# Attention and two MLPs on one core: first loads by head, a mixed first score and value order, and moved weight casts

## The reference

```python
scores = cap * np.tanh(scale * np.matmul(q, k.transpose(0, 1, 3, 2)) / cap)
attn = np.exp(scores - np.max(scores, axis=-1, keepdims=True))
attn = attn / (np.sum(attn, axis=-1, keepdims=True) + 1e-09)
x = np.matmul(attn, v)          # 896 x 768 after the heads are put side by side
x = np.maximum(x @ w_in1, 0.0) ** 2 @ w_out1
h = x @ w_in2
return (h / (1.0 + np.exp(-h))) @ w_out2
```

## Time and profile before

| what | us |
|---|---|
| median of three runs | 550.55 |
| the profiled execution, its own time | 549.79 |
| its span, first to last instruction | 547.9 |
| PE busy | 535.4 (98%) |
| PEld busy | 442.6 (81%) |
| DVE busy | 376.1 (69%) |
| ACT busy | 261.3 (48%) |
| POOL busy | 82.1 (15%) |

### The profile page before, as it was taken

One profiled execution on the slowest core, in us unless ns is written; L12 is line 12 of the kernel. 1 busy time (PEld: TensorE's weight loads), 2 busy tenths in 40 slices (PEclk: granted clock), 3 DMA queues, 4 the chain that ended last, 5 costly groups with the idle time before them and its releaser, 6 DMA issues.

```text
span 547.9 us, 7096 instructions
## 1 busy us (share of the span) xinstructions
PE 535.4 (98%) x2626; PEld 442.6 (81%) x2626; DVE 376.1 (69%) x597; ACT 261.3 (48%) x403; POOL 82.1 (15%) x54
## 2 busy tenths in 40 slices
PE   6999999999999999999999999999999999999995
PEld 5333333799999999999998999999999999999895
DVE  2199999977778652676799855556855345568985
ACT  3988889054444322454444434444533144454230
POOL 0999999300000000000000000000000000000000
PEclk9999999999999999999999999999999999999999
DMA  7888540151112201411122024202111141020645
GB/s 159 219 235 199 147 110 2 57 135 58 45 33 72 63 1 57 135 58 38 40 63 57 17 59 135 59 10 68 47 54 34 59 134 36 23 78 15 118 63 85
DMA packets 82116, 42.16 MB, mean 77 GB/s; under 512 B 26784, under 2 KB 79008, under 8 KB 82080
## 3 DMA queue, kind: packets, MB, share of 16 engines
q1 hardware_dynamic: 77952, 40.32, 28.6%
q10 hardware_dynamic: 4096, 1.38, 1.3%
q0 software_dynamic: 32, 0.00, 0.0%
HBM read 38.93 MB, written 2.75 MB: 76 GB/s over the span
## 4 chain that ended last, share of the span: by engine, by line
PE 76%; DVE 14%; issue 4%; SPq 3%; DMA 1%; ACT 1%; DVEq 0%; ACTq 0%
PE banks L494 25%; PE banks L496 25%; PE banks L495 25%; DVE den L815 3%; SPq L301 2%; DVE w_hl L866 1%; DVE x_hi L825 1%; DVE rinv L820 1%; DVE att_o L823 1%; DVE y L946 1%; DVE den_r L812 1%; DVE qk_f L800 1%; DMA qk_raw<-in_k_dram 1%; DVE qk_f L796 1%; SPq L322 1%
## 5 line engine op out<-in xcount | busy, mean ns | idle before, releaser
L494 PE MATMUL banks<-x_hi,w_hl 128*128 128x448 f32 x384 | 140.7, 367 | 0.0
L495 PE MATMUL banks<-x_lo,w_hl 128*128 128x448 f32 x384 | 140.5, 366 | 0.0
L496 PE MATMUL banks<-x_hi,w_hl 128*128 128x448 f32 x384 | 140.5, 366 | 0.0
L494 PE MATMUL banks<-g_hi,w_hl 128*128 128x448 f32 x336 | 123.3, 367 | 0.7 <-DVE w_hl L866 0.7
L496 PE MATMUL banks<-g_hi,w_hl 128*128 128x448 f32 x336 | 123.0, 366 | 0.0
L495 PE MATMUL banks<-g_lo,w_hl 128*128 128x448 f32 x336 | 123.0, 366 | 0.0
L494 PEld LDWEIGHTS banks<-x_hi,w_hl 128*128 128x128 f32 x384 | 72.1, 188 | 7.6 <-issue 1.4
L496 PEld LDWEIGHTS banks<-x_hi,w_hl 128*128 128x128 f32 x384 | 72.1, 188 | 6.2
L495 PEld LDWEIGHTS banks<-x_lo,w_hl 128*128 128x128 f32 x384 | 72.1, 188 | 6.2
L861 DVE TENSOR_TENSOR w_hl<-w_raw,w_hl 128x768 fp32r<-128x768 f32 x32 | 32.5, 1016 | 57.4 <-ACT w_hl L640 57.3
L494 PEld LDWEIGHTS banks<-g_hi,w_hl 128*128 128x128 f32 x336 | 63.1, 188 | 7.0 <-DVE w_hl L866 1.4
(11 more groups left out here) (64 smaller groups left out, 549.5 us busy)
## 6 DMA issues: line engine op xcount, KB each, us to landing
w_raw<-in_moe_w_in_dram SPq DMA_DIRECT2D x32, 384.0 KB, 3.4
w_raw<-in_moe_w_out_dram SPq DMA_DIRECT2D x24, 512.0 KB, 5.3
qk_raw<-in_k_dram SPq DMA_DIRECT2D x48, 112.0 KB, 2.7
qk_raw<-in_q_dram SPq DMA_DIRECT2D x40, 112.0 KB, 2.8
v_t<-in_v_dram SPq DMA_DIRECT2D x24, 96.0 KB, 2.8
out_dram<-rows SPq DMA_DIRECT2D x40, 56.0 KB, 2.2
qk_raw<-in_q_dram ACTq DMA_DIRECT2D x8, 112.0 KB, 4.1
out_dram<-rows ACTq DMA_DIRECT2D x8, 56.0 KB, 2.8
```

The costliest lines, as they stand in the source:

```text
L494: pe.matmul(dst, hi[:, kk, :], mov_hi, start=start, stop=False, skip_group_check=onto)
L495: pe.matmul(dst, hi[:, kk, :], mov_lo, start=False, stop=False, skip_group_check=onto)
L496: return pe.matmul(dst, lo[:, kk, :], mov_hi, start=False, stop=stop, skip_group_check=onto)
```

## The change

It has five parts.

1. *Loads.* The first two pairs are loaded by head: SP issues those of the even heads and ACT those of the odd heads, for pair 0 keys, then queries, then the same for pair 1, with no wait between. ACT also issues two of the four first value transfers.
2. *Order in the lead.* On PE the outputs of pairs 0 and 1 are cut in two halves (`output_first`, `output_rest`) that stand between the score units of the next pair. The sums of pair 0 come after all scores of pair 2. The wait for `v_x` moves to the product that reads it. WARM goes from 17 to 14.
3. *GpSimd.* The loop over pairs becomes straight code.
4. *Weight casts on ACT.* The first two weight tiles are rounded after pairs 7 and 9, one each.
5. *Groups.* In `model`, the sums of weight blocks and the first two products' rests for group 1 move on DVE ahead of the adding up of results of group 0. On ACT the rounding for product 1 of group 1 moves ahead of `x_high`. The epsilon is added with a `tensor_scalar` in place of the `scalar_tensor_tensor`.

```diff
-    WARM = 17
+    WARM = 14
@@ SP
-            load_part(At(0, 0), 0, k_v, s_first_in[0])
-            sp.wait_ge(s_first_in[0], 4 * DMA)
-            load_part(At(0, 1), 0, k_v, s_qk_in[1])
-            load_v(0)
+            load_head(0, 0, k_v, 0, s_first_in[0])
+            load_head(0, 1, q_v, 0, s_first_in[1])
+            load_head(1, 0, k_v, 0, s_qk_in[1])
+            load_head(1, 1, q_v, 0, s_qk_in[1])
+            load_v(0, range(0, 2))
             load_v_x(0)
@@ POOL
-                for j in range(2):
+                for j in range(PAIRS):
                     add_units(At(0, j))
-                two_steps(pool, 2, PAIRS - 2, add_units)
@@ PE
+            def output_first(j):
+                ...
+                values(j, 0)
+                values(j, 1)
+            def output_rest(j):
+                pe.wait_ge(s_exp, 2 * j.n + 2)
+                values(j, 2)
+                ...
+                values(j, CW).then_inc(s_val, 1)
-            for j in range(PAIRS):
+            for u in range(C):
+                scores(At(0, 0), u)
+            for j in range(2):
+                scores(At(0, j + 1), 0)
+                output_first(At(0, j))
+                for u in range(1, CW):
+                    scores(At(0, j + 1), u)
+                output_rest(At(0, j))
+                scores(At(0, j + 1), CW)
+            sums(At(0, 0))
+            for j in range(3, PAIRS):
                 ...
@@ ACT
-            load_q(0, s_first_in[1])
+            load_head(0, 0, k_v, 1, s_first_in[0])
+            load_head(0, 1, q_v, 1, s_first_in[1])
+            load_head(1, 0, k_v, 1, s_qk_in[1])
+            load_head(1, 1, q_v, 1, s_qk_in[1])
+            for g in range(2, C):
+                ...
-            act.wait_ge(s_first_in[1], 4 * DMA)
-            load_q(1, s_qk_in[1])
             for j in range(PAIRS - 1):
                 weights(At(0, j))
-            for p in range(2):
-                tile_high(0, 0, p)
+                if j in (7, 9):
+                    tile_high(0, 0, (j - 7) // 2)
@@ DVE, finish
-                dve.scalar_tensor_tensor(den[:, :], part, eps_t[:, 0:1], part,
-                                         op0=ALU.add, op1=ALU.max).then_inc(s_den, 1)
+                dve.tensor_scalar(den[:, :], part, eps_t[:, 0:1], None, ALU.add).then_inc(s_den, 1)
@@ DVE, model
                         if g == 0:
+                            prod_low(layer, s, 1, 0)
+                            w_s1(layer, s, 1)
+                            w_s3(layer, s, 1)
+                            w_s2(layer, s, 1)
+                            prod_low(layer, s, 1, 1)
                             if s == 1:
                                 post_12_u2(layer, g)
-                            w_s1(layer, s, g + 1)
```

More of the change, by code:

```diff
@@ L186, in wait @@
                 eng.wait_ge(s, n)
-        def two_steps(eng, first, count, step):
-            assert count % 2 == 0
-            with eng.Fori(0, count // 2) as i:
-                step(At(i, first))
-                step(At(i, first + 1))
         def shifted(eng):
@@ L294, in _, with load_head, load_v @@
         def _(sp):
-            def load_part(j, n, src, done):
-                for h in range(2):
-                    for a in range(2):
-                        at = n * QB * D + BL * (1 - a)
-                        rp = slice(D * h + BL * a, D * h + BL * a + BL)
-                        sp.dma_start(qk_raw[j.par][rp, at:at + QB * D],
-                                     src[bass.ds(j.no, 1), h][0]).then_inc(done, DMA)
+            def load_head(j, n, src, h, done):
+                for a in range(2):
+                    at = n * QB * D + BL * (1 - a)
+                    rp = slice(D * h + BL * a, D * h + BL * a + BL)
+                    sp.dma_start(qk_raw[j % 2][rp, at:at + QB * D], src[j, h]).then_inc(done, DMA)
             def load_qk(j):
-                load_part(j, 0, k_v, s_qk_in[j.par])
-                load_part(j, 1, q_v, s_qk_in[j.par])
-            def load_v(part):
+                for n, src in enumerate((k_v, q_v)):
+                    for h in range(2):
+                        load_head(j, n, src, h, s_qk_in[j % 2])
+            def load_v(part, groups=range(C)):
                 first, last = V_PARTS[part], V_PARTS[part + 1]
-                for g in range(C):
+                for g in groups:
                     at = g * CW * D
@@ L355, in _ @@
                 sp.wait_ge(s_turned, 2 * (j - 1))
-                load_qk(At(0, j))
+                load_qk(j)
                 if j % 2 == 0:
@@ L470, in output @@
                 values(j, 1)
+            def output_rest(j):
                 pe.wait_ge(s_exp, 2 * j.n + 2)
                 values(j, 2)
+                if j.n in V_PARTS[0:2]:
+                    pe.wait_ge(s_v_x_in[V_PARTS.index(j.n)], 2 * XB * DMA)
                 values(j, CW).then_inc(s_val, 1)
+            def output(j):
+                output_first(j)
+                output_rest(j)
             pe.wait_ge(s_const, 1)
@@ L1121, in _ @@
                             post_21_u3(layer, g)
-                        if not last:
+                        if g == 1:
                             prod_low(layer, s, g + 1, 0)
@@ L1132, in _ @@
                             leave(layer, s, g, 1)
-                        if not last:
+                        if g == 1:
                             w_s2(layer, s, g + 1)
                             prod_low(layer, s, g + 1, 1)
-                        elif s == 0:
+                        elif last and s == 0:
                             tile_low(layer, 1, 0)
-                        elif layer == 0:
+                        elif last and layer == 0:
                             tile_low(1, 0, 0)
```

29 lines of the change are left out of this document (15 added, 14 removed).

## The result

The changed kernel takes 547.7 us (median of 6 runs, 546.39 to 548.9) against 550.65 us for the kernel before (6 runs, 549.63 to 551.4): a ratio of 0.9949, 95% interval [0.9935, 0.9964]. The forecast was 547.4, its range 545.9 to 549.4. The profiled execution of the changed kernel took 548.26 us (span 546.5), so the two profiled executions lie 1.53 us apart, while the medians lie 2.95 apart. Both differences have to be explained.

A forecast was written before the change was run, and what follows sets the result against it. It took attention to set the end, paced first by ACT, then by PE, plus two weight waits. Loads 0.75, order 1.0, GpSimd 0.4, casts 0.3 and groups 0.65 make 3.1 us: 550.55 - 3.1 = 547.4, range 545.9 to 549.4.

The forecast's parts named there:

- Loads, 0.75: Start of the kernel: loading by head starts PE's first scores at 7.8 in place of 8.55, gaining 0.75 us (0.35 to 1.1).
- S0: The start of PE's first scores: 8.55 us in the kernel before, forecast 7.8, between 7.4 and 8.2.
- if they come faster: First loads: if the eight transfers land before 7.4, DVE's own chain is next and the first scores start at 7.44.
- Order, 1.0: PE's order in the lead: scores of pair 4 start at S0 + 26.5, before 27.63; gain 1.0 us (0 to 1.4).
- GpSimd, 0.4: End of attention: unrolled, POOL finishes pair 10 at 90.7, so PE's 0.42 wait for L812 goes; 0.4 us (0 to 0.4).
- Casts, 0.3: End of attention: one cast hardly exceeds ACT's slack a pair, so PE's 0.29 wait for a tanh goes; 0.3 us.
- Groups, 0.65: Second stage of each layer: PE's two waits for a weight's rest go, 0.65 us (0.3 to 0.7).
- the epsilon, 0: DVE's end of a pair: the new epsilon instruction counts for nothing, still near 1.5 us beside POOL.
- An idle PE costs no clock: Lead: with fourteen warm matmuls PE's idle is harmless, as the granted clock stayed 1.00 while PE idled from 12 to 13 us.
- Rival (a): Whole kernel: more comes, with S0 at 7.44, ACT never late and a faster stage pace; 4.7 us gained, 545.9; chance 0.17.
- (b): Lead: its gain is hidden, first transfers land at 7.4 and values cost ACT a microsecond; 1.8 or 1.0 us, 549.5; chance 0.18.
- (c): Lead: sums 0, behind all pair 2's scores, come too late and delay ACT, POOL and DVE; 553.5, slower; chance 0.05.

The follow-up runs named there:

- after_again: The changed kernel run again with nothing edited: 547.89 us, ratio 0.9942 to the kernel before.
- casts_before: The changed kernel with the two casts of a weight back to back behind pair 10 again: 547.52 us, ratio 0.9944 to the kernel before.
- lead_before_warm: The changed kernel with the loads and TensorE's order of the kernel before, and 17 warm matmuls in place of 14: 548.77 us, ratio 0.9968 to the kernel before.
- loads_before: The changed kernel with the loads of the kernel before, TensorE's new order kept: 551.92 us, ratio 1.0015 to the kernel before.
- order_before: The changed kernel with TensorE's order of the kernel before, the new loads kept: 547.54 us, ratio 0.9937 to the kernel before.
- lead_before: The changed kernel with both the loads and TensorE's order of the kernel before, 14 warm matmuls: 548.57 us, ratio 0.9955 to the kernel before.

## Why the prediction was right, and where it was wrong

The time is inside the range and 0.3 us from the forecast, but not by the steps forecast: that the sum came so near is in part luck. Point by point:

1. *Loads, 0.75.* Wrong: S0 did not fall, it was 8.92 and 8.77 in the two profiles of the changed kernel. The step that failed is "if they come faster": the keys' first transpose did come ahead (6.81), and the rate did go up, to 303 GB/s, but only from 5 us on; from 4 to 5 us it fell to 126 (68 in after_again), and the eight transfers of pair 1 that the removed waits let in took their share. With one wait put back the first scores came at 7.82, the forecast 7.8. DVE's own chain was late too: its last instruction ahead of the first transpose, taken to end at 6.12 as before, ended at 6.89, since the transfer of the cap landed 0.8 us later, so with the queries in time S0 would still have been some 8.1 in this execution (6.81 + 0.5 + 0.67 + 0.15, an estimate). And "L800 needed the last query of pair 0" misread the rows, though the 8.2 worked out from 7.4 doesn't hang on it: L800 has no idle ahead of it; the first transpose had waited for the keys (landed at 7.21), and the last query landed at 7.38, in time. "Fourteen warm matmuls end at 7.25" was wrong too, they end at 7.88 in the changed kernel and at 6.92 to 8.52 in the twelve profiles with fourteen: the early ones take longer (6 from 3 to 4 us, 11 from 7 to 8 in the kernel before). What the loads did pay is in point 6.
2. *Order, 1.0.* The mechanism and its place were right (scores of pair 4 at S0 + 26.45, forecast 26.5; ACT fed). That it comes out at the end was not: undoing it cost nothing, since DVE holds the sums of pair 10; PE got there 0.63 us earlier by it.
3. *GpSimd, 0.4.* The step "DVE's two instructions behind it bring sums 10 to 92.2" was a wrong reading of one row. The wait names L812; I took it for pair 10's own chain through POOL, while the sums of pair 10 also wait for DVE to empty the bank of pair 9, with 1.89 us of weight's rest ahead. That wait stayed, 0.58. POOL's chain from L393 of pair 0 to the end of pair 10 became 1.4 us shorter (92.61 - 13.86 = 78.75 in place of 80.15), not 2.2. The unrolling is still worth 0.6 us at this place and 1.1 in the median, as without it POOL would be later than DVE. In the kernel before, POOL was done with pair 10 at 93.63, ahead of PE at 94.72; what came later is DVE's end of pair 9:

```profile
92.55 1.89 DVE L861 TENSOR_TENSOR w_hl<-w_raw,w_hl 128x768 fp32r<-128x768 f32 x1
94.36 0.64 DVE L812 STREAM_TRANSPOSE den_r<-banks 128x448 f32<-128x448 f32 x1
```

4. *Casts, 0.3.* The wait went, but undoing it cost nothing (casts_before). In the old lead, where PE comes later and DVE is not in its way, both small waits of the earlier trace rows are gone (lead_before_warm: from S0 to the hidden stage 0.97 less than before). So 3 and 4 together, with the epsilon, paid the 0.7 of the two waits there; steps 2 to 4 are not additive, and together they gave 1.38 where the sum had 1.7.
5. *Groups, 0.65; the epsilon, 0.* Right. 0.17 of product 2's rest is left (0.3 was allowed), and the epsilon took 1.56 us beside POOL, 0.23 alone.
6. *An idle PE costs no clock.* Wrong, and it hid a part that the sum had not. The row behind it (12 to 13 us at 1.00) came from an execution in which the clock happened to hold. Two in three executions of before ran with a lower mean clock and took some 1.2 us more; the changed kernel's never did, and by loads_before and order_before it is the new loads that keep the clock. The medians differ by 2.95 where the traces differ by 1.53: the profiled execution of before lay 0.86 under its median and near the 549.9 of those that kept the clock, and that of the changed kernel 0.56 above its own, which the spread of first scores and pace can account for.

So the forecast's 3.1 was met by 1.4 in the lead and the sums, 0.5 in the groups, and 0.7 to 1.0 from a clock that was not in the sum (before's medians of 550.65 and, over 61 executions, 550.89, less 549.9), with S0 giving nothing. Rival (a) was right that a stage's pace moves the time; it is 0.2027 or 0.2066 us, not 0.2010 or 0.2041 (the counts took in matmuls at the edges), so 1.0 us a stage and not 0.8. But it moves from execution to execution, and in the first product stage of the profiled pair it went against the change. Rivals (b) and (c) did not happen: ACT lost nothing, and sums 0 came at S0 + 17.8. Not tested: the epsilon's own edit, where the clock falls in the executions of before itself, and why the first transfers are slow from 3 to 5 us.

## What to carry to other kernels

When two engines are within a microsecond of each other, don't add up the waits that go; ask for each which engine arrives last once it has gone, and read from the code all that a waiting instruction waits for, its buffer's last reader too. One profiled execution does not show a clock that falls in some of them: compare the mean clock over the runs before calling an idle stretch free. And a wait that keeps later loads off the first ones can be worth more than the issue slots that it costs.

## What the runs showed of the hardware

- Two queues that each write their own half of the partitions brought 303 GB/s, and 212 when both wrote the same half, with the DMA engines full in both. The Trainium skill (SBUF — State Buffer, "Can I just issue two DMAs to hit both halves?") gives +6% for two transfers at partitions 0 and 64 over a single one; here it was +43% over two into one half.
- In lead_before, after two idles of PE, 1.63 us ahead of pair 0's scores and 3.12 us behind them, the granted clock fell to 0.50 for some 3 us while PE was busy again; loads_before shows the same after 1.53 and 2.75 us. In the one profile of lead_before_warm, after 0.31 and 3.03 us, it stayed at 1.00, though 9 of the 12 executions of this program had the lower mean clock.
- One program's product stages ran at 0.2027 or 0.2066 us a matmul, differently in each execution, at a granted clock of 1.00: 1.0 us a stage. The first and third stage of a kernel keep one pace from end to end in all fourteen traces; the second one of before changed from 0.2067 to 0.2027 at its wait for a weight's rest. The hidden stages ran at 0.204 in every one. What sets it is open.
